# Storing the last block with one transfer per unit, and splitting two units' transposes over several steps, in an attention and feed-forward kernel

## Chip, cores and metric

The kernel runs on 1 core of one Trainium2 chip. The metric is device time in microseconds (us) of one execution; lower is better. TensorE is called PE, VectorE DVE, ScalarE ACT, GpSimd POOL and SyncE SP, as in the profile; SPq and ACTq are the queues on which SP and ACT issue transfers.

## What is computed

```python
def _attn_ref(r, k, v, w, u):              # B=4, H=8, S=768, D=48
    for t in range(S):
        kt, vt, rt = (k[:, :, t], v[:, :, t], r[:, :, t])
        cur = np.einsum('bhd,bhe->bhde', u[None] * kt, vt)
        y[:, :, t] = np.einsum('bhd,bhde->bhe', rt, state + cur)
        state = w[None, :, :, None] * state + np.einsum('bhd,bhe->bhde', kt, vt)
# x = y laid out as 3072 tokens x 384
def _moe_ref(x, w_in, w_out):              # 384 -> 2048 -> 384
    g = np.maximum(x @ w_in, 0.0) ** 2
    return g @ w_out
def _moe2_ref(x, w_a, w_b, w_out):         # 384 -> 1536 -> 384
    return ((x @ w_a) * (x @ w_b)) @ w_out
```

All in float32. Each product of matrices in the two feed-forward layers is made of three passes on PE (high part by high part, high by low, low by high).

## The kernel before

The 3072 tokens are 6 blocks of 512. A block is 4 units of attention (24 in all, numbered `e`); a unit is 2 batches by 64 time steps, 128 rows. The first block's attention is made at the start. From then on the attention of block m is made beside layer 1 of block m-1. Layer 1 of a block has 16 steps; a step's global number is `s = n * 16 + f`. In step s, PE multiplies `up` for step s+2, then does what stands beside the step (a `mix` of a unit, if one is placed there), then `down` for step s. DVE in step s squares the hidden values of step s+2 (`square`), does the placed work, and makes their low part `g_lo` (`square_lo`). All orders are written out by hand: `place` puts units at steps by a table, and each engine's `layer1` asks at each step what stands there.

A unit needs on DVE: its k transposed and scaled (`flip_k`), its r transposed and scaled (`flip_r`), a sum for the diagonal (`sum_diagonal`, for which POOL makes the products), and later `mask` and `keep_state`. Units 8 and up are transposed on DVE; earlier ones on PE. `flip_k` has one buffer `kT`, so it waits until PE has scored the unit before. `mix(e, s)` on PE waits for both scalings of unit e+1, runs `mix_state`, then waits for `g_lo` of step s+1 and scores unit e+1, then runs two more groups.

Before the change, unit 8 is placed at step 8, where unit 6 is mixed: `flip_k` follows `keep_state`, `flip_r` stands at the step's end, and the sum at step 9. Unit 9 is placed at step 13, in which nothing is mixed: `flip_k` and `flip_r` both stand ahead of `square`, and the sum behind it. `mix(8)` stands at step 14.

The kernel's end: in layer 2 of the last block the last step's products finish in four chunks of PSUM, one per 128 tokens, each counted by `chunk_done`. Each chunk is copied to `y_out` in SBUF (128 partitions by 384 floats), chunks 0 and 2 by ACT, 1 and 3 by DVE, and stored by `store_unit`. The 128 partitions of a chunk are 64 tokens of one batch and 64 of another, so its rows lie in two places of the result. SP stores chunks 0, 1 and 2 in this order, ACT chunk 3; each as two transfers of 64 rows. SP then waits for all of them. The stores of the earlier blocks (L480) are 4 transfers of 192 KB each, whose outermost dimension is 64.

Of the kernel before, what the change touches and what calls it, by code (L numbers as in the profile page):

```python
# [28 lines left out]
def attention_ffn_kernel(nc, r, k, v, w, u, w_in, w_down, w_a, w_b, w_out, out):  # L29
# [5 lines left out]
    T = HP  # L35
# [28 lines left out]

    TURN, LATER, FLIP, SCORE, MIX, SPLIT = range(6)
    beside = [{} for _ in range(6)]

    def place(m, turns, later, mixes, splits):  # L70
        for i in range(UNITS):
            e, start = m * UNITS + i, (m - 1) * N1
            beside[FLIP if e >= FLIPPED else LATER if i in later else TURN][start + turns[i]] = e

            assert mixes[i] % 2 == 0
            beside[MIX][start + mixes[i]] = e
            beside[SPLIT].setdefault(start + splits[i], []).append(e)

    beside[SCORE][3] = UNITS
    place(1, [2, 3, 5, 7], [1, 2, 3], [4, 6, 8, 10], [9, 11, 12, 12])  # L80
    for m in range(2, BLOCKS):
        place(m, [-8, -3 if m == 2 else -4, 1 if m == 2 else 0, 4], [], [-2, 2, 6, 10], [5, 6, 12, 12])

    MAIN = 2 * D
# [12 lines left out]
    with ctx:  # L98
# [3 lines left out]
        def sem(name):  # L102
            return ctx.enter_context(nc.semaphore(name))
# [132 lines left out]
        acc_read, x2_stored = sem("acc_read"), sem("x2_stored")  # L236
        x2_loaded = [sem(f"x2_loaded{i}") for i in range(2)]
        up2_done, chunk_done, y_stored = sem("up2_done"), sem("chunk_done"), sem("y_stored")
        even_out, odd_out = sem("even_out"), sem("odd_out")

        def after(eng, signal, count):
            if count > 0:
# [141 lines left out]

        def store_unit(eng, e):

            for i in range(2):
                eng.dma_start(out_t[2 * i + e % 2, LAST, :, e // 2, :], y_out[i * T:(i + 1) * T, e, :])\
                    .then_inc(y_stored, 16)

        block = ctx.enter_context(nc.Block())

        @block.sync
        def _(sp):
            def load_half(e):
                sp.wait_ge(mixed, e - 2)
                load_rk(sp, e, 1, k, k_loaded)
                load_rk(sp, e, 0, r, r_loaded)
                load_v(sp, e)

            def blocks_free(e):

                if e == FLIPPED:

                    sp.wait_ge(scored, UNITS)
                    sp.wait_ge(rest_zeroed, 1)
                    sp.wait_ge(choice_made, 1)
                elif e == FLIPPED + 2:

                    after_split(sp, N1 - 2)  # L410
                    sp.wait_ge(r_flipped, 1)
                elif e == FLIPPED + 4:
                    after_split(sp, N1 - 1)
                else:
                    sp.wait_ge(k_flipped, e - 2 - FLIPPED)
                    sp.wait_ge(r_flipped, e - 2 - FLIPPED)

            def store_x2(n):
                sp.wait_ge(acc_read, (n + 1) * KT)
                sp.dma_start(x2_dram[n, :, :], x2_flat).then_inc(x2_stored, 16)  # L420

            def load_x2(n):
                sp.wait_ge(x2_stored, 16 * (n + 1))
                sp.dma_start(xT[:, n % 2, LO, :, :].rearrange("p k t -> p (k t)").bitcast(F32),
                             x2_dram[n, :, :]).then_inc(x2_loaded[n % 2], 16)

            for e in (0, 2):
                load_rk(sp, e, 1, k, k_loaded)
                load_rk(sp, e, 0, r, r_loaded)
            for e in (0, 2):  # L430
                load_v(sp, e)
            for i in range(2):
                load_weights(sp, i)
            repack(sp, 0)
            for i in range(2, STAGES + 1):
                load_weights(sp, i)

            sp.wait_ge(y_mixed, UNITS)
            load_half(UNITS)
            load_half(UNITS + 2)  # L440
            blocks_free(FLIPPED)
            load_blocks(sp, FLIPPED)

            for n in range(BLOCKS):
                if n > 0:
                    store_x2(n - 1)
                if n < LAST:
                    for e in range((n + 1) * UNITS, (n + 2) * UNITS, 2):
                        repack(sp, e)
                        if e + UNITS < ALL:  # L450
                            load_half(e + UNITS)
                        if e == FLIPPED - 2:
                            blocks_free(FLIPPED + 2)
                            load_blocks(sp, FLIPPED + 2)
                        if FLIPPED + 2 < e + UNITS + 2 < ALL:
                            blocks_free(e + UNITS + 2)
                            load_blocks(sp, e + UNITS + 2)
                if n == LAST - 1:
                    sp.wait_ge(k_flipped, ALL - FLIPPED)
                    sp.wait_ge(r_flipped, ALL - FLIPPED)  # L460
                    for i in range(N1, N1 + STAGES):
                        load_weights(sp, i)

            sp.wait_ge(up_done, N1 * LAST)
            load_x2(0)
            for i in range(N1 + STAGES, N1 + N2):
                load_weights(sp, i)
            sp.wait_ge(up_done, N1 * BLOCKS)
            load_x2(1)
            store_x2(LAST)  # L470

            for n in range(BLOCKS):
                if 1 <= n < LAST:
                    sp.wait_ge(up2_done, n * 2 * N2)
                    load_x2(n + 1)
                if n < LAST:
                    sp.wait_ge(acc_read, BLOCKS * KT + (n + 1) * UNITS)
                    for p in range(2):
                        for i in range(2):
                            sp.dma_start(out_t[2 * i + p, n, :, :, :], y_out[i * T:(i + 1) * T, p::2, :])\  # L480
                                .then_inc(y_stored, 16)

            sp.wait_ge(even_out, 1)
            store_unit(sp, 0)
            sp.wait_ge(odd_out, 1)
            store_unit(sp, 1)
            sp.wait_ge(even_out, 2)
            store_unit(sp, 2)
            sp.wait_ge(y_stored, 16 * (4 * LAST + 2 * UNITS))

        @block.gpsimd
        def _(pool):
# [405 lines left out]
        def _(act):  # L898
# [118 lines left out]
            def take_out(n):  # L1017
                after(act, y_stored, n * 4 * 16)
                if n == 0:
                    act.wait_ge(x2_stored, 16 * BLOCKS)  # L1020
                if n == LAST:

                    for b in (0, 2):
                        act.wait_ge(chunk_done, b + 1)
                        nc.scalar.activation(y_out[:, b, :], acc2[b][:, 0:DM], ACT.Copy).then_inc(even_out, 1)
                    act.wait_ge(odd_out, 2)
                    store_unit(act, 3)
                    return
                act.wait_ge(down_done, STEPS1 + (n + 1) * N2)
                for b in range(UNITS):  # L1030
                    nc.scalar.activation(y_out[:, b, :], acc2[b][:, 0:DM], ACT.Copy).then_inc(acc_read, 1)
# [16 lines left out]
        def _(dve):  # L1048
# [162 lines left out]
            def layer1(n):  # L1211
                for f in range(N1):
                    ahead = (n, f + 2) if f + 2 < N1 else (n + 1, f + 2 - N1) if n < LAST else None
                    s = n * N1 + f

                    flip_first = s in beside[FLIP] and s not in beside[MIX]
                    if flip_first:
                        flip_k(beside[FLIP][s])
                        flip_r(beside[FLIP][s])
                    if ahead:  # L1220
                        square(*ahead)
                    if flip_first:
                        sum_diagonal(beside[FLIP][s])
                    if s - 1 in beside[FLIP] and s - 1 in beside[MIX]:
                        sum_diagonal(beside[FLIP][s - 1])
                    if s in beside[TURN]:
                        sum_diagonal(beside[TURN][s])
                        scale(beside[TURN][s])
# [2 lines left out]
                    if s in beside[MIX]:  # L1231
                        e = beside[MIX][s]
                        if e + 1 < ALL:
                            mask(e + 1)
                        if e < LEAVING:
                            keep_state(e)
                        if s in beside[FLIP]:
                            flip_k(beside[FLIP][s])
                    if ahead:
                        square_lo(*ahead)  # L1240
                    if s in beside[LATER]:
                        scale(beside[LATER][s])
                        sum_diagonal(beside[LATER][s])
# [3 lines left out]
                        x2_lo(0, f - 8)  # L1247
                    for i in split_beside(n, f):
                        split_lo(nc.vector, i)
                    if s in beside[FLIP] and not flip_first:  # L1250
                        flip_r(beside[FLIP][s])

            dve.wait_ge(rest_zeroed, 1)
            for e in range(2):
# [59 lines left out]
                    if n < LAST and 4 <= j < 4 + KT:  # L1314
                        x2_lo(n + 1, j - 4)
            dve.wait_ge(y_stored, LAST * 4 * 16)
            for b in (1, 3):
                dve.wait_ge(chunk_done, b + 1)
                nc.vector.tensor_copy(y_out[:, b, :], acc2[b][:, 0:DM]).then_inc(odd_out, 1)

# [21 lines left out]
```

## Time and profile before

| | |
|---|---|
| median of 3 runs | 918.14 us (917.87 to 919.39) |
| profiled execution, its own time | 918.38 us |
| its span in the trace | 916.6 us |
| PE busy, share of the span | 906.4 us, 99% |
| DVE, ACT, POOL busy | 43%, 31%, 13% |
| DMA, read and written | 38.54 MB and 9.44 MB, mean 52 GB/s |

Times in the trace are from the span's start. The chain of work that ended last is PE for 95% of the span. The tail is what comes after PE's last matmul: copies, issues, data, the landing. The "DMA share" is the mean busy share of 16 DMA engines.
### The profile page before, as it was taken

How to read it: one execution, taken by the hardware profiler on the slowest of the kernel's cores; microseconds unless marked ns; L12 is line 12 of the kernel's file. 1: busy time of each engine (PE TensorE's matmuls, PEld its weight loads, DVE VectorE, ACT ScalarE, POOL GpSimd, SP SyncE). 2: the span in 40 equal slices, each digit the busy share in tenths (PEclk: the TensorE clock that was granted, in tenths of full speed). 3: DMA queues.
4: the chain of work that ended last, by engine and by line, in shares of the span. 5: the costliest groups of instructions: out<-in, count | busy, mean ns of one | idle time of the engine just before them, and what ended most of it. 6: DMA issues, size and time to landing. Idle time of an engine off the chain costs nothing.

```text
span 916.6 us, 16503 instructions
## 1 busy us (share of the span) xinstructions
PE 906.4 (99%) x6951; PEld 774.9 (85%) x6951; DVE 390.8 (43%) x600; ACT 286.0 (31%) x501; POOL 122.7 (13%) x125
## 2 busy tenths in 40 slices
PE   8999999999999999999999999999999999999997
PEld 6888888888888888888888888888888888888886
DVE  8778655546555555336542212322321222222122
ACT  3434333333333233344542222212222222222121
POOL 7355322232223221000000000000000000000000
PEclk9999999999999999999999999999999999999999
DMA  9987536635435320043330001002002002001001
GB/s 154 176 141 144 92 55 118 93 76 86 79 64 92 54 64 20 18 131 120 93 105 1 1 12 59 1 1 70 0 1 69 1 1 69 1 1 34 1 1 35
DMA packets 175800, 53.39 MB, mean 58 GB/s; under 512 B 147949, under 2 KB 174190, under 8 KB 175726
## 3 DMA queue, kind: packets, MB, share of 16 engines
q1 hardware_dynamic: 168832, 47.41, 25.7%
q10 hardware_dynamic: 6894, 4.92, 2.5%
q8 instruction: 55, 0.90, 0.4%
q14 instruction: 19, 0.16, 0.1%
HBM read 38.54 MB, written 9.44 MB: 52 GB/s over the span
## 4 chain that ended last, share of the span: by engine, by line
PE 95%; DVE 1%; issue 1%; POOL 1%; ACT 0%; ACTq 0%; POOLq 0%; DVEq 0%
PE banks L850 11%; PE banks L852 11%; PE banks L851 11%; PE banks L736 7%; PE banks L737 7%; PE banks L740 7%; PE banks L720 7%; PE banks L722 7%; PE banks L721 7%; PE banks L864 5%; PE banks L868 5%; PE banks L865 5%; PE banks L638 1%; PE banks L651 1%; PE banks L618 1%
## 5 line engine op out<-in xcount | busy, mean ns | idle before, releaser
L1298 DVE TENSOR_TENSOR g_raw<-banks,g_raw 128x512 f32<-128x512 f32 x72 | 49.8, 692 | 277.0 <-PE banks L852 277.0
L850 PE MATMUL banks<-xT,weights 128*128 128x512 f32 x360 | 140.2, 389 | 0.0
L851 PE MATMUL banks<-xT,weights 128*128 128x512 f32 x360 | 140.0, 389 | 0.0
L852 PE MATMUL banks<-xT,weights 128*128 128x512 f32 x360 | 140.0, 389 | 0.0
L736 PE MATMUL banks<-g_hi,weights 128*128 128x512 f32 x288 | 114.8, 398 | 0.0
L1183 DVE TENSOR_TENSOR g_lo<-banks,g_hi 128x512 fp32r<-128x512 f32 x94 | 65.1, 692 | 113.1 <-ACT g_hi L912 113.1
L720 PE MATMUL banks<-xT,weights 128*128 128x512 f32 x288 | 112.4, 390 | 0.0
L737 PE MATMUL banks<-g_hi,weights 128*128 128x512 f32 x288 | 112.2, 390 | 0.0
L721 PE MATMUL banks<-xT,weights 128*128 128x512 f32 x288 | 112.1, 389 | 0.0
L722 PE MATMUL banks<-xT,weights 128*128 128x512 f32 x288 | 112.0, 389 | 0.0
L912 ACT ACTIVATE g_hi<-banks 128x512 fp32r<-128x512 f32 x94 | 56.4, 600 | 150.2 <-PE banks L740 107.9
L1012 ACT ACTIVATE g_raw<-banks 128x512 f32<-128x512 f32 x72 | 43.1, 598 | 168.7 <-PE banks L852 168.7
L1015 ACT ACTIVATE g_hi<-g_raw 128x512 fp32r<-128x512 f32 x72 | 45.5, 632 | 160.6 <-DVE g_raw L1298 160.6
L1178 DVE TENSOR_TENSOR banks<-banks,g_raw 128x512 f32<-128x512 f32 x94 | 65.4, 696 | 51.0 <-ACT g_raw L906 50.8
L906 ACT ACTIVATE g_raw<-banks 128x512 f32<-128x512 f32 x96 | 57.4, 598 | 84.9 <-PE banks L722 83.1
L864 PE MATMUL banks<-weights,g_hi 128*128 128x384 f32 x240 | 80.9, 337 | 0.0
L740 PE MATMUL banks<-g_lo,weights 128*128 128x512 f32 x288 | 80.9, 389 | 0.0
L865 PE MATMUL banks<-weights,g_hi 128*128 128x384 f32 x240 | 80.6, 336 | 0.0
L852 PEld LDWEIGHTS banks<-xT,weights 128*128 128x128 f32 x360 | 67.6, 188 | 14.2
L850 PEld LDWEIGHTS banks<-xT,weights 128*128 128x128 f32 x360 | 67.6, 188 | 11.7
L851 PEld LDWEIGHTS banks<-xT,weights 128*128 128x128 f32 x360 | 67.6, 188 | 11.7
L1301 DVE TENSOR_TENSOR g_lo<-g_raw,g_hi 128x512 fp32r<-128x512 f32 x72 | 49.8, 692 | 50.3 <-ACT g_hi L1015 50.3
(131 smaller groups left out, 1246.6 us busy)
## 6 DMA issues: line engine op xcount, KB each, us to landing
rkv<-in_v SPq DMA_DIRECT2D x24, 192.0 KB, 4.4
x_dram<-stage SPq DMA_DIRECT2D x6, 768.0 KB, 3.4
xT<-x_dram SPq DMA_DIRECT2D x6, 768.0 KB, 5.5
result<-stage SPq DMA_DIRECT2D x20, 192.0 KB, 3.0
xT<-y_pad SPq DMA_DIRECT2D x22, 144.0 KB, 2.8
stage<-in_moe_w_out SPq DMA_DIRECT2D x16, 192.0 KB, 3.2
rkv<-in_k SPq DMA_DIRECT2D x12, 192.0 KB, 3.6
rkv<-in_k SPq DMA_DIRECT2D x24, 96.0 KB, 3.6
```

The lines of the kernel that those rows point to most:

```text
L720: nc.tensor.matmul(hid[f % 2][:, :], hi, xT[:, q, HI, kt, :], start=(kt == 0), stop=False)
L721: nc.tensor.matmul(hid[f % 2][:, :], hi, xT[:, q, LO, kt, :], start=False, stop=False)
L722: last = nc.tensor.matmul(hid[f % 2][:, :], lo, xT[:, q, HI, kt, :], start=False, stop=(kt == KT - 1))
L736: nc.tensor.matmul(acc[m][:, :], hi(m), g_hi[:, f % 2, :], start=(f == 0), stop=False)
L737: nc.tensor.matmul(acc[m][:, :], lo(m), g_hi[:, f % 2, :], start=False, stop=False)
L740: last = nc.tensor.matmul(acc[m][:, :], hi(m), g_lo[:, f % 2, :], start=False, stop=(f == N1 - 1))
L850: nc.tensor.matmul(dst, hi, xT[:, q, HI, kt, :], start=(kt == 0), stop=False)
L851: nc.tensor.matmul(dst, hi, xT[:, q, LO, kt, :], start=False, stop=False)
L852: last = nc.tensor.matmul(dst, lo, xT[:, q, HI, kt, :], start=False, stop=(kt == KT - 1))
L864: nc.tensor.matmul(acc2[b][:, 0:DM], p_hi, hi, start=(j == 0), stop=False)
L865: nc.tensor.matmul(acc2[b][:, 0:DM], p_hi, lo, start=False, stop=False)
L1178: nc.vector.tensor_tensor(squared(n, f), squared(n, f), g_raw[:, f % 2, :], ALU.mult)\
```

## The change

Two parts. First, `store_unit` issues one transfer for a unit in place of two; its destination takes both batches by a stride of 2 in the outermost dimension. ACT now copies chunks 0 and 3, DVE chunks 1 and 2, and the last store, by ACT's queue, waits for ACT's own copy. Second, `flip_k`, `flip_r` and the sum get a table each for units 8 and 9: unit 8 has `flip_k` at step 8, `flip_r` and the sum at step 9; unit 9 has `flip_k` at step 10, `flip_r` at step 12, the sum at step 13. Units 10 and up stay where they were.

```diff
+            if e in (FLIPPED, FLIPPED + 1):
+                for kind, at in zip((FLIP_K, FLIP_R, SUM), turns[i]):
+                    beside[kind][start + at] = e
...
-    for m in range(2, BLOCKS):
-        place(m, [-8, -3 if m == 2 else -4, 1 if m == 2 else 0, 4], [], [-2, 2, 6, 10], [5, 6, 12, 12])
+    place(2, [(-8, -7, -7), (-6, -4, -3), 1, 4], [], [-2, 2, 6, 10], [5, 6, 12, 12])
+    for m in range(3, BLOCKS):
+        place(m, [-8, -4, 0, 4], [], [-2, 2, 6, 10], [5, 6, 12, 12])
...
         def store_unit(eng, e):
-            for i in range(2):
-                eng.dma_start(out_t[2 * i + e % 2, LAST, :, e // 2, :], y_out[i * T:(i + 1) * T, e, :])\
-                    .then_inc(y_stored, 16)
+            eng.dma_start(out_t[e % 2::2, LAST, :, e // 2, :], y_out[:, e, :]).then_inc(y_stored, 16)
...
-            sp.wait_ge(even_out, 1)
+            sp.wait_ge(outer_out, 1)
             store_unit(sp, 0)
-            sp.wait_ge(odd_out, 1)
+            sp.wait_ge(inner_out, 1)
             store_unit(sp, 1)
-            sp.wait_ge(even_out, 2)
+            sp.wait_ge(inner_out, 2)
             store_unit(sp, 2)
-            sp.wait_ge(y_stored, 16 * (4 * LAST + 2 * UNITS))
+            sp.wait_ge(y_stored, 16 * (4 * LAST + UNITS))
...
-                    for b in (0, 2):
+                    for b in (0, 3):
                         act.wait_ge(chunk_done, b + 1)
-                        nc.scalar.activation(y_out[:, b, :], acc2[b][:, 0:DM], ACT.Copy).then_inc(even_out, 1)
-                    act.wait_ge(odd_out, 2)
+                        nc.scalar.activation(y_out[:, b, :], acc2[b][:, 0:DM], ACT.Copy).then_inc(outer_out, 1)
+                    act.wait_ge(outer_out, 2)
                     store_unit(act, 3)
...
-                    flip_first = s in beside[FLIP] and s not in beside[MIX]
-                    if flip_first:
+                    if s in beside[FLIP]:
                         flip_k(beside[FLIP][s])
                         flip_r(beside[FLIP][s])
                     if ahead:
                         square(*ahead)
-                    if flip_first:
+                    if s in beside[FLIP]:
                         sum_diagonal(beside[FLIP][s])
-                    if s - 1 in beside[FLIP] and s - 1 in beside[MIX]:
-                        sum_diagonal(beside[FLIP][s - 1])
+                    if s in beside[FLIP_R]:
+                        flip_r(beside[FLIP_R][s])
...
-                        if s in beside[FLIP]:
-                            flip_k(beside[FLIP][s])
+                    if s in beside[FLIP_K]:
+                        flip_k(beside[FLIP_K][s])
                     if ahead:
                         square_lo(*ahead)
+                    if s in beside[SUM]:
+                        sum_diagonal(beside[SUM][s])
...
-                    if s in beside[FLIP] and not flip_first:
-                        flip_r(beside[FLIP][s])
...
-            for b in (1, 3):
+            for b in (1, 2):
                 dve.wait_ge(chunk_done, b + 1)
-                nc.vector.tensor_copy(y_out[:, b, :], acc2[b][:, 0:DM]).then_inc(odd_out, 1)
+                nc.vector.tensor_copy(y_out[:, b, :], acc2[b][:, 0:DM]).then_inc(inner_out, 1)
```

How the instructions of DVE stand from step 12 to step 13, before (L1178 is `square`, L1183 `square_lo`, L1201 the low part of the next block's input, L1139 and L1141 `flip_k`, L1146 and L1148 `flip_r`, L1108 the sum):

```order
L1178 TENSOR_TENSOR banks<-banks,g_raw 128x512
L1183 TENSOR_TENSOR g_lo<-banks,g_hi 128x512
L1201 TENSOR_TENSOR xT<-xT 128x3x128 x2
L1139 STREAM_TRANSPOSE kT<-stage 128x512
L1141 TENSOR_TENSOR kT<-kT,pow_down 112x512
L1146 STREAM_TRANSPOSE rT<-stage 128x512
L1148 TENSOR_TENSOR rT<-rT,pow_up 112x512
L1178 TENSOR_TENSOR banks<-banks,g_raw 128x512
L1108 TENSOR_REDUCE diag<-rku 128x8
L1183 TENSOR_TENSOR g_lo<-banks,g_hi 128x512
```

The same two steps in the changed kernel, whose lines are numbered 5 higher there (L1183 is now `square`, L1188 `square_lo`, L1206 the input's low part, L1151 and L1153 `flip_r`, L1113 the sum):

```order
L1183 TENSOR_TENSOR banks<-banks,g_raw 128x512
L1151 STREAM_TRANSPOSE rT<-stage 128x512
L1153 TENSOR_TENSOR rT<-rT,pow_up 112x512
L1188 TENSOR_TENSOR g_lo<-banks,g_hi 128x512
L1206 TENSOR_TENSOR xT<-xT 128x3x128 x2
L1183 TENSOR_TENSOR banks<-banks,g_raw 128x512
L1188 TENSOR_TENSOR g_lo<-banks,g_hi 128x512
L1113 TENSOR_REDUCE diag<-rku 128x8
```

Unit 9's `flip_k` has left this stretch (it stands at step 10, behind `keep_state`), its `flip_r` has moved up by one step into the place between `square` and `square_lo`, and the sum stands behind `square_lo`.

The end of SP's queue before, with the waits (L388 is in `store_unit`; the sizes are those of the destination, outermost first):

```order
L480 DMA result<-stage 64x2x384 x3
L388 DMA result<-stage 64x384 [waits even_out]
L388 DMA result<-stage 64x384
L388 DMA result<-stage 64x384 [waits odd_out]
L388 DMA result<-stage 64x384
L388 DMA result<-stage 64x384 [waits even_out]
L388 DMA result<-stage 64x384
L98 UNCONDITIONAL_BRANCH [waits y_stored]
```

The same in the changed kernel:

```order
L485 DMA result<-stage 64x2x384 x3
L394 DMA result<-stage 2x64x384 [waits outer_out]
L394 DMA result<-stage 2x64x384 [waits inner_out] x2
L105 UNCONDITIONAL_BRANCH [waits y_stored]
```

Six issues have become three, and the outermost dimension of the destination was 64 and is 2; the source's, the partitions, was 64 and is 128. ACT's queue goes in the same way from two issues of 64x384 to one of 2x64x384. At ACT's start stands the one other transfer with few outermost entries that the text below speaks of, in both kernels:

```order
L968 DMA y_pad<-in_w 4x2x48
L970 DMA y_pad<-in_u 1x384
L972 ACT_TABLE_LOAD
```

The first of these writes 4 partitions with 2 pieces of 48 floats each; it moves nothing between the two kernels.

## Rows read from the trace of the kernel before

**Rows 1.** The page, busy time of the engines, share of the span.

```profile
PE 906.4 (99%) x6951; PEld 774.9 (85%) x6951; DVE 390.8 (43%) x600; ACT 286.0 (31%) x501; POOL 122.7 (13%) x125
```

**Rows 2.** Waits of PE from 60 us on: total us, times, longest.

```profile
PE banks L618 <- DVE g_lo L1183: 0.4, 1, 0.4
```

**Rows 3.** Timeline of PE: start, us, instruction, idle before it.

```profile
95.30 0.39 PE L720 MATMUL banks<-xT,weights 128*128 128x512 f32 x1
...
102.78 0.84 PE L740 MATMUL banks<-g_lo,weights 128*128 128x512 f32 x3
...
106.62 0.69 PE L618 MATMUL banks<-rT,kT 48*64 48x64 f32 x32 [0.36 <-DVE g_lo L1183]
```

**Rows 4.** Timeline of DVE, steps 8 to 13.

```profile
80.65 1.78 DVE L1141 TENSOR_TENSOR kT<-kT,pow_down 112x512 f32<-112x512 f32 x1
...
92.11 0.69 DVE L1183 TENSOR_TENSOR g_lo<-banks,g_hi 128x512 fp32r<-128x512 f32 x1 [1.39 <-ACT g_hi L912]
...
100.28 0.69 DVE L1183 TENSOR_TENSOR g_lo<-banks,g_hi 128x512 fp32r<-128x512 f32 x1 [1.36 <-ACT g_hi L912]
100.88 1.02 DVE L1201 TENSOR_TENSOR xT<-xT 128x384 fp32r<-128x384 f32 x2
101.82 0.71 DVE L1139 STREAM_TRANSPOSE kT<-stage 128x512 f32<-128x512 f32 x1
...
104.52 0.69 DVE L1178 TENSOR_TENSOR banks<-banks,g_raw 128x512 f32<-128x512 f32 x1
...
105.87 0.69 DVE L1183 TENSOR_TENSOR g_lo<-banks,g_hi 128x512 fp32r<-128x512 f32 x1 [0.21 <-ACT g_hi L912]
```

**Rows 5.** Timelines of POOL and of ACT in the same stretch.

```profile
80.88 1.01 POOL L517 TENSOR_TENSOR rku<-rkv,u_rows 128x384 f32<-128x384 f32 x1
...
101.62 0.60 ACT L906 ACTIVATE g_raw<-banks 128x512 f32<-128x512 f32 x1 [0.56 <-PE banks L722]
```

**Rows 6.** Timelines of the last microseconds: ACT and its queue, DVE, SP's queue.

```profile
911.27 0.49 ACT L1025 ACTIVATE stage<-banks 128x384 f32<-128x384 f32 x1 [0.49 <-PE banks L868]
912.38 1.21 ACTq L388 DMA_DIRECT2D result<-stage  x2
...
911.79 0.56 DVE L1319 COPY stage<-banks 128x384 f32<-128x384 f32 x1 [0.42 <-PE banks L868]
...
910.80 3.73 SPq L388 DMA_DIRECT2D result<-stage  x6
```

**Rows 7.** DMA from 911.6 us on, in windows: width, busy engines, PEclk, DMA share, GB/s.

```profile
911.60:912.00 0.40, 0.15 (x1) 0.00 (x0) 0.21 (x1) 0.16 (x1) 0.00 (x0) 1.00 0.11 27
...
915.60:915.80 0.20, 0.00 (x0) 0.00 (x0) 0.00 (x0) 0.00 (x0) 0.00 (x0) 1.00 0.31 100
915.80:916.00 0.20, 0.00 (x0) 0.00 (x0) 0.00 (x0) 0.00 (x0) 0.00 (x0) 1.00 0.00 0
```

**Rows 8.** DMA packets from 910 to 917 us, the eight stores of 64 rows.

```profile
DMA packets 640, 0.79 MB, mean 112 GB/s; under 512 B 128, under 2 KB 640, under 8 KB 640
```

**Rows 9.** DMA to 3.4 us: packets of ACT's queue; the transfer of w, its KB.

```profile
q10 hardware_dynamic: 12, 0.00, 0.3%
...
y_pad<-in_w ACTq DMA_DIRECT2D x1, 1.5 KB
```

**Rows 10.** The four stores of 192 KB of the block before (L480), 843.5 to 848.6 us.

```profile
DMA packets 576, 0.79 MB, mean 154 GB/s; under 512 B 64, under 2 KB 576, under 8 KB 576
...
q1 hardware_dynamic: 576, 0.79, 56.3%
```

**Rows 11.** When SP issued them: start, us for all.

```profile
843.51 2.54 SPq L480 DMA_DIRECT2D result<-stage  x4
```

**Rows 12.** The same stores in windows of 0.4 us, columns as in Rows 7.

```profile
846.20:846.60 0.40, 0.40 (x4) 0.40 (x4) 0.40 (x1) 0.00 (x0) 0.00 (x0) 1.00 0.87 215
...
847.40:847.80 0.40, 0.40 (x4) 0.40 (x4) 0.40 (x1) 0.00 (x0) 0.00 (x0) 1.00 1.01 376
847.80:848.20 0.40, 0.40 (x3) 0.33 (x2) 0.22 (x1) 0.00 (x0) 0.00 (x0) 1.00 0.28 92
```

More of the change, by code:

```diff
@@ L62, in attention_ffn_kernel @@
     assert LATE_SIZE >= LATE * TILE2 and (N2 - LATE) * TILE2 <= N1 * 2 * W1
-    TURN, LATER, FLIP, SCORE, MIX, SPLIT = range(6)
-    beside = [{} for _ in range(6)]
+    TURN, LATER, FLIP, FLIP_K, FLIP_R, SUM, SCORE, MIX, SPLIT = range(9)
+    beside = [{} for _ in range(9)]
     def place(m, turns, later, mixes, splits):
@@ L72, in place @@
             e, start = m * UNITS + i, (m - 1) * N1
-            beside[FLIP if e >= FLIPPED else LATER if i in later else TURN][start + turns[i]] = e
+            if e in (FLIPPED, FLIPPED + 1):
+                for kind, at in zip((FLIP_K, FLIP_R, SUM), turns[i]):
+                    beside[kind][start + at] = e
+            else:
+                beside[FLIP if e >= FLIPPED else LATER if i in later else TURN][start + turns[i]] = e
             assert mixes[i] % 2 == 0
@@ L238, in attention_ffn_kernel @@
         up2_done, chunk_done, y_stored = sem("up2_done"), sem("chunk_done"), sem("y_stored")
-        even_out, odd_out = sem("even_out"), sem("odd_out")
+        outer_out, inner_out = sem("outer_out"), sem("inner_out")
         def after(eng, signal, count):
```

## The prediction

> **What bounds the kernel now.** I read the page first: PE is busy for 906.4 of 916.6 us [rows 1], so a change can only win what PE waits for, or what lies after its last matmul. Then the list of PE's waits from 60 us on, where all of the changed schedule lies: it has one entry, 0.36 us [rows 2, 3]. That is the score of unit 9 inside `mix(8)`, which was ready at 106.26 us and started at 106.62 because `g_lo` of step 15 came late. The timeline of DVE shows why. DVE finished the last work of step 12 late (L1201, 100.88 to 101.9), then put `flip_k` and `flip_r` of unit 9 (101.82 to 104.52, 2.70 us) ahead of `square`, though ACT had the input of `square` ready at 102.22; so `g_lo` started at 105.87 and ended at 106.56 [rows 4, 5]. Last the tail, from timelines and narrow windows: ACT's queue is through with its two issues at 913.59, SP's with its six at 914.53, 3.73 us after the first at 910.80, some 0.62 us each [rows 6]. The first data moves at about 911.9, the last at about 915.8, and the span ends 0.8 us later [rows 7]. The tail is set by SP's issues: chunk 2 is copied at 911.76, but the last issue starts some 2.1 us later [rows 6].
>
> **Part 1, the transposes.** Nothing is added; five instructions of unit 9 and three of unit 8 move. At step 12, `flip_r` of unit 9 falls into DVE's idle 1.36 us between `square` and the `g_lo` of 100.28; a pair of transpose and scaling takes half of 2.70, 1.35 us, so it fits [rows 4]. At step 10, `flip_k` falls into an idle 1.39 us in the same way [rows 4]. At step 13 `square` now starts at about 102.3, and not 104.52; ACT's high part waits for it and for PE's `down` of step 13, which ends at 103.62 [rows 3]; from there `g_lo` is done no later than the 1.35 us by which its start followed `square`'s before, 105.0, some 1.2 us ahead of the score at 106.26. So PE's 0.36 us go. What lies queued behind `flip_k` at step 10 is that step's `g_lo` (92.11); PE needs it for the `up` that starts at 95.30 [rows 3, 4], so 2.5 us of cover. Unit 8 moves its `flip_r` behind `square` instead of ahead of it, which frees `g_lo` of that step and leaves the mix at step 10 on time. Bounds: one scaling of this form took 1.78 us beside POOL's products, against 0.69 as a rule [rows 4, 5]; if `flip_k` at step 10 meets the same, its step is 1.1 us later, inside the cover. So this part is worth between 0 (the lateness is handed on) and 0.4; I take **-0.36 us**.
>
> **Part 2, the stores.** Issues: SP has three in place of six, so its queue is through at about 910.80 + 3 x 0.62 = 912.7, ACT's store is issued at about 912.3 after its own copy of 0.49 us [rows 6]. On its face that takes 1.8 us off SP's queue. But a transfer must be dealt out to DMA engines, and here the shape matters. The stores of 64 rows show 640 packets for 8 transfers: 8 x 64 = 512 of data and 128 of under 512 bytes, which is 16 closing packets for each, so 16 engines [rows 8]. The four stores of 192 KB, whose outermost dimension is 64 too, show 512 + 64, again 16 each [rows 10]. The transfer of w has 4 outermost entries. It is 1.5 KB in pieces of 48 floats (192 bytes), which is 8 packets of data, and there are 12 packets: 4 closing ones, so 4 engines [rows 9]. The trace thus shows that few outermost entries mean few engines. The new stores have 2 outermost entries in the destination and 128 in the source. No row shows a transfer whose two sides differ so. I take it that the smaller side decides, since each engine must be given a whole slice of both sides: **2 engines** for each store, and I take it to be the same two for all four.
>
> The Trainium skill says just this: in "DMA: Bandwidth & Descriptors", section "Why a DMA increments its semaphore by 16 and not by 1", the number of engines is the largest up to 16 that divides the outermost non-1 size of both sides, and they are the lowest-numbered ones. The trace agrees in its three countable cases, none of them with unequal sides.
>
> The price: 4 stores x 128 rows over 2 engines are 256 packets for each engine. A packet's time from the stores of the block before: at their fastest 376 GB/s over 16 engines at a share of 1.01, 1536 x 16 / 376 = 65 ns; in slow windows 215 GB/s, 1536 x 16 / 215 = 114 ns [rows 12]; in the mean 0.563 x 5.1 x 16 / 512 = 90 ns [rows 10]. That one and the same kind of packet takes 65 or 114 ns while all engines are busy says that the slow ones wait for something the 16 share; two engines alone move at most 47 GB/s, so I take the fast end, 65 ns: 256 x 0.065 = **16.7 us** (23.0 at the mean, 29.2 at the slow pace).
>
> **Sum**, in the profiled execution. First data at 911.9 - 0.36 = 911.5; last at 911.5 + 16.7 = 928.2; the span's end 0.8 later, 929.0; against 916.6 that is +12.4. What lies outside the span (918.38 - 916.6 = 1.8 us) stays. The profiled time is 0.24 us above the median of the runs, 918.14, so I add the difference to the median: 918.14 + 12.4 = **930.6 us**. Own range of this case: from 926.4, if ACT's store has engines of its own and SP's three take 3 x 64 x 0.065 = 12.5 us, to 943.1 at 114 ns. I keep 925 to 941, as two lone engines should be nearer to the fast rows. The swapped copies (ACT 0.49 us, DVE 0.56) cost or give less than 0.1 us beside this.
>
> **Rivals.**
> 1. *Sixteen engines all the same* (the side with 128 partitions decides, or the transfer is cut otherwise). For it: the stores whose source has 64 partitions run on 16 [rows 8, 10], and no row tells which side is asked. Then the tail is like the stores of the block before: four transfers of 192 KB issued 0.6 us apart, whose data ended between 847.8 and 848.2, about 4.6 us after the first issue at 843.51 [rows 11, 12]. Here 910.80 + 4.6 = 915.4 against 915.8: -0.4, and up to 0.3 more because ACT issues the fourth at 912.3 beside SP. It would not give the 1.8 us of issue time, since the DMA engines become the bound. With -0.36 that is -0.8 to -1.1: 917.0 to 917.4 us, no change that can be measured (0.2% is 1.8 us here, about what a measurement of this kernel can tell from no change). The Trainium skill's table in "Rules for kernel authors" of the same page even asks for one transfer of 128 partitions in place of two over halves; it takes both to run on all engines, which is this rival. Chance 0.13.
> 2. *Two engines, each queue with its own pair*: 926.4 us as above. Against it: nothing in the trace tells queues' engines apart. Inside the forecast's range, chance 0.05.
> 3. *Two engines at the mean pace or slower*, if the pace is that of writing rows from far-apart partitions and not of sharing: 90 ns give 911.5 + 23.0 + 0.8 - 916.6 = +18.7, so 936.8 us. For it: 90 ns is the mean of the row [rows 10]; against it: two lone engines share with nobody. Chance 0.2, inside the range up to about 108 ns.
> 4. *The schedule makes a new wait*: if a `flip_r` of unit 8 or 9 also took 1.78 us, it would end 1.1 us later; the mix at step 10 would wait up to 0.4 us, an estimate from that 1.1 us less the 0.7 us that I count as cover there. That changes the sum by less than 1 us, and would turn the sign only where the first rival holds and the mix waits over 1.1 us. Chance 0.1, beside any of the others.
>
> **How the numbers follow.** Two engines 0.83 (0.2 of it at a slower pace, 0.05 with pairs apart), sixteen 0.13, a number in between (4 or 8, 920 to 924 us) 0.04. The predicted time is that of two engines at 65 ns. The range 925 to 941 holds 0.83 less 0.03 for a pace above 108 ns: 0.80. Slower by over 0.2%: 0.83 + 0.04 = 0.87, less a little for a number in between that hides, 0.86. Of the sixteen-engine case, 0.11 within 0.2% and 0.03 faster, if both queues overlap better than the row of the block before.
>
> **What would show it.** In the changed kernel's trace: PE without a wait from 60 us on, score of unit 9 at about 106.3; `square` of step 13 at about 102.3. In the tail SPq with three issues ended by 912.7, and then a DMA share of about 2/16 = 0.12 at some 47 GB/s, for 16 to 17 us; 520 packets for the four stores (512 + 8), where sixteen engines would give 576. The long wait would be SP's last, for `y_stored`. The prediction is wrong if the count is 576, and only its size is wrong if the share is 0.12 but the GB/s differ from 47.

## The result, and the profile after

The changed kernel takes 931.18 us in the median of 4 runs (930.15 to 931.94), against 918.0 us before in the same comparison: a ratio of 1.014, 95% interval 1.0122 to 1.0157. The predicted time was 930.6 us, slower with a chance of 0.86.

The page of the changed kernel first, busy time and share of the span, against [rows 1]:

```profile
span 930.2 us, 16499 instructions
...
PE 906.5 (97%) x6951; PEld 774.5 (83%) x6951; DVE 391.6 (42%) x600; ACT 286.1 (31%) x501; POOL 122.4 (13%) x125
```

No engine works longer; the span is 13.6 us longer, and PE's share falls to 97%. So the time lies after PE. The list of SP's waits from 905 us on says where:

```profile
SPq L394 <- ACT stage L1030: 64.7, 1, 64.7
SPq L105 <- DMA result<-stage: 14.3, 1, 14.3
```

The same wait in the kernel before:

```profile
SPq L98 <- DMA result<-stage: 1.7, 1, 1.7
```

The wait at the program's end, for the last stores, is 14.3 us and was 1.7. The timelines of the tail, SP's queue, ACT and its queue, DVE, against [rows 6]:

```profile
911.36 4.09 SPq L394 DMA_DIRECT2D result<-stage  x3
...
912.35 0.49 ACT L1030 ACTIVATE stage<-banks 128x384 f32<-128x384 f32 x1 [1.01 <-PE banks L873]
912.87 0.61 ACTq L394 DMA_DIRECT2D result<-stage  x1
...
911.38 1.02 DVE L1323 COPY stage<-banks 128x384 f32<-128x384 f32 x2 [1.13 <-PE banks L873]
```

The last of the four issues to start is ACT's, at 912.87 us. SP's third starts at 912.60 and takes 2.85 of the 4.09 us, so it ends at 915.45; the two before it took 0.62 and 0.52. The DMA packets from 910 to 931 us, against [rows 8]:

```profile
DMA packets 520, 0.79 MB, mean 37 GB/s; under 512 B 8, under 2 KB 520, under 8 KB 520
...
q1 hardware_dynamic: 390, 0.59, 8.1%
q10 hardware_dynamic: 130, 0.20, 2.5%
```

q1 is SP's queue and q10 ACT's; the numbers are packets, MB and the share of the 16 engines' time. There are 512 rows and 8 closing packets for 4 stores: 2 engines each, where 16 closed each store before. DMA in windows, columns as in [rows 7]:

```profile
914.00:916.00 2.00, 0.00 (x0) 0.00 (x0) 0.00 (x0) 0.00 (x0) 0.00 (x0) 1.00 0.13 38
916.00:918.00 2.00, 0.00 (x0) 0.00 (x0) 0.00 (x0) 0.00 (x0) 0.00 (x0) 0.62 0.13 51
918.00:920.00 2.00, 0.00 (x0) 0.00 (x0) 0.00 (x0) 0.00 (x0) 0.00 (x0) 0.50 0.13 49
...
929.00:929.50 0.50, 0.00 (x0) 0.00 (x0) 0.00 (x0) 0.00 (x0) 0.00 (x0) 0.50 0.12 43
929.50:930.20 0.70, 0.00 (x0) 0.00 (x0) 0.00 (x0) 0.00 (x0) 0.00 (x0) 0.50 0.00 0
```

The share is 0.13, which is 2 of 16 engines. From 918 to 922 us each of the two queues moved 66 packets at this share: the queues share one pair. They move 49 to 51 GB/s: 2 x 1536 bytes each 61 ns. After ACT's copy ends at 912.84 us no engine computes any more; only the issues and the data are left. (The last column but two is the clock granted to PE, whose last matmul ended at 912.3 us. It reads 0.50, the lower of its two levels, from 918 us on.)

From the first issue to the span's end the tail is 930.2 - 911.36 = 18.8 us, before it was 916.6 - 910.80 = 5.8: +13.0 us. The first issue itself comes 0.56 us later than before. To see why, I follow PE's products with `g_lo` (L740 before, L745 after), one group for each step of layer 1. Each row is the group of one step of the changed kernel, 9 to 14:

```profile
85.02 0.84 PE L745 MATMUL banks<-g_lo,weights 128*128 128x512 f32 x3
...
91.25 0.85 PE L745 MATMUL banks<-g_lo,weights 128*128 128x512 f32 x3
...
95.36 0.84 PE L745 MATMUL banks<-g_lo,weights 128*128 128x512 f32 x3
...
99.85 0.84 PE L745 MATMUL banks<-g_lo,weights 128*128 128x512 f32 x3
...
103.93 0.84 PE L745 MATMUL banks<-g_lo,weights 128*128 128x512 f32 x3
...
110.12 0.84 PE L745 MATMUL banks<-g_lo,weights 128*128 128x512 f32 x3
```

The same groups of before start at 84.11, 90.52, 94.62, 98.70, 102.78 and 109.56. So this execution is 0.91 us late at step 9. It was so at step 8 too (80.94 against 80.03 us), ahead of the moved work, so this is the timing of its start. At step 14 it is 0.56 us late. From step 9 to step 14 it takes 25.10 us in place of 25.45: -0.35. Step by step the distances are 6.23, 4.11, 4.49, 4.08, 6.19, and before 6.41, 4.10, 4.08, 4.08, 6.78. Two steps with a mix became shorter, by 0.18 and 0.59 us, and one step longer, by 0.41. From step 14 to the first store both take 801.24 us.

### The profile page after: what moved, and what is told of

It reads as the page before. It is cut to its first block, busy times and chain, and to the rows that moved or that the text cites. A ratio compares the mean times of both kernels' runs of the same rounds, so it can differ in the third digit from the quotient of the medians.

```text
span 930.2 us, 16499 instructions
## 1 busy us (share of the span) xinstructions
PE 906.5 (97%) x6951; PEld 774.5 (83%) x6951; DVE 391.6 (42%) x600; ACT 286.1 (31%) x501; POOL 122.4 (13%) x125
## 4 chain that ended last, share of the span: by engine, by line
PE 92%; SPq 3%; DVE 2%; DMA 1%; issue 0%; POOL 0%; ACT 0%; ACTq 0%; DVEq 0%
PE banks L855 11%; PE banks L857 11%; PE banks L856 11%; PE banks L741 7%; PE banks L742 7%; PE banks L745 7%; PE banks L725 7%; PE banks L726 7%; PE banks L727 7%; PE banks L869 5%; PE banks L873 5%; PE banks L870 5%; PE banks L643 1%; PE banks L656 1%; PE banks L623 1%; SPq L329 1%
## 5 line engine op out<-in xcount | busy, mean ns | idle before, releaser
L1188 DVE TENSOR_TENSOR g_lo<-banks,g_hi 128x512 fp32r<-128x512 f32 x94 | 65.0, 691 | 111.5 <-ACT g_hi L917 111.5
L1183 DVE TENSOR_TENSOR banks<-banks,g_raw 128x512 f32<-128x512 f32 x94 | 65.4, 696 | 51.0 <-ACT g_raw L911 50.8
L745 PE MATMUL banks<-g_lo,weights 128*128 128x512 f32 x288 | 80.9, 389 | 0.0
```

Of the source, the lines that this page charges most:

```text
L745: last = nc.tensor.matmul(acc[m][:, :], hi(m), g_lo[:, f % 2, :], start=False, stop=(f == N1 - 1))
L1183: nc.vector.tensor_tensor(squared(n, f), squared(n, f), g_raw[:, f % 2, :], ALU.mult)\
```

## The experiments

Each ratio is taken to runs of the kernel before that were made beside it; their medians are 918.26 to 918.62 us.

**Each part alone.** Kernel one is that of before with the new end (DVE copies chunks 1 and 2, and the waits follow, as in the change):

```diff
-            for i in range(2):
-                eng.dma_start(out_t[2 * i + e % 2, LAST, :, e // 2, :], y_out[i * T:(i + 1) * T, e, :])\
-                    .then_inc(y_stored, 16)
+            eng.dma_start(out_t[e % 2::2, LAST, :, e // 2, :], y_out[:, e, :]).then_inc(y_stored, 16)
...
-                    for b in (0, 2):
+                    for b in (0, 3):
```

> The kernel before with only the end of the changed kernel: one transfer of 2x64x384 for each unit, chunks 0 and 3 copied by ACT. If the whole loss is from two outermost entries, thus two DMA engines: 520 packets in the four stores, DMA share 0.13 at about 49 GB/s for some 16.9 us, 931.2 us plus or minus 0.8 (the time of the changed kernel, plus up to 0.4 for PE's old wait at the score of unit 9). If part of the loss is from the moved transposes: at least 1 us less than the changed kernel, under 930 us.

Measured: 931.38 us (930.86 to 931.77), 1.0142 of before (1.0126 to 1.0157). 520 packets again; its tail is 929.5 - 910.67 = 18.8 us. PE's wait at the score of unit 9 is there (0.35 us). With the transposes as before the loss is all there: it comes from the new end.

Kernel two has the new tables and `layer1` of DVE, and the stores, copies and waits of before.

> The kernel before with only the moved transposes. If the stores are the whole loss: 917.3 to 918.3 us, same as before. In the trace PE's 0.36 us wait at the score of unit 9 is gone. In the changed kernel PE started the product up for step 14 some 0.4 us late (at 96.28 us), just after DVE's low part of weight tile 14 ended (96.22). If that is caused by the unit's k scaled at step 10 ahead of it, the same gap stands here; if it came from the later start of that execution alone, it doesn't.

Measured: 917.91 us (917.04 to 918.69), 0.9995 of before (0.9985 to 1.0004), no change that can be told. From step 9 to 14 it takes 24.68 us, 0.77 less than before, and no wait of PE is left in the list. Here PE's late start at step 12 was 0.04 us, not 0.41.

**Where the destination lies.** In the changed kernel, only the destination of the four stores differs. This kernel's result is not the right one, as the rows of the last block stand permuted in it; it only answers the question:

```diff
-            eng.dma_start(out_t[e % 2::2, LAST, :, e // 2, :], y_out[:, e, :]).then_inc(y_stored, 16)
+            rows = out.rearrange("(b c t) d -> b c t d", b=B, c=BLOCKS)
+            eng.dma_start(rows[e, LAST, :, :], y_out[:, e, :]).then_inc(y_stored, 16)
```

> The changed kernel, but each of the last four stores writes its 128 rows to one place of the result (128 rows in a row, outermost 128, so that rows of the last block stand permuted in the result). One transfer for a unit stays. If the outermost entries of the destination set the number of engines: 576 packets, all 16 engines, the tail like the four 192 KB stores of the block before, last data some 4.6 us after the first issue, 916.9 to 917.8 us. If one transfer of 128 partitions is slow by itself (many rows behind one issue), it stays near 931 us.

Measured: 916.01 us (915.34 to 916.61), 0.9973 of before (0.9964 to 0.9983). Its packets, and three of its windows, columns as in [rows 7]:

```profile
DMA packets 576, 0.79 MB, mean 30 GB/s; under 512 B 64, under 2 KB 576, under 8 KB 576
...
911.43:911.83 0.40, 0.00 (x0) 0.00 (x0) 0.00 (x0) 0.00 (x0) 0.00 (x0) 1.00 1.03 369
911.83:912.23 0.40, 0.00 (x0) 0.00 (x0) 0.00 (x0) 0.00 (x0) 0.00 (x0) 1.00 1.05 373
912.23:912.63 0.40, 0.00 (x0) 0.00 (x0) 0.00 (x0) 0.00 (x0) 0.00 (x0) 1.00 1.03 365
```

16 closing packets for each store: all engines. With the same source, queues and number of rows, the destination alone makes 15 us. Two things differ in it, the outermost size (128 for 2) and the number of places (1 for 2); the next kernel tells them apart. It also came out 0.9 us under my expectation: it moves at 365 to 373 GB/s, while the first store of 64 rows before, when alone, moved at 207:

```profile
912.00:912.20 0.20, 0.00 (x0) 0.00 (x0) 0.20 (x1) 0.00 (x0) 0.00 (x0) 1.00 0.85 207
```

That is taken up below.

It gives each store 4 places of 32 rows (permuted rows again):

```diff
+            rows = out.rearrange("(b c q t) d -> b c q t d", b=B, c=BLOCKS, q=UNITS)
+            eng.dma_start(rows[:, LAST, e, :, :], y_out[:, e, :]).then_inc(y_stored, 16)
```

> The changed kernel, but each of the last four stores writes 4 places of 32 rows (outermost 4; rows of the last block stand permuted in the result). If the number of engines is that of the destination's outermost entries: 512 + 16 = 528 packets, DMA share about 0.25 at some 98 GB/s, 512 / 4 x 61 ns = 7.8 us of data in place of 15.6, so 922.5 to 924.5 us. If only two places far apart are slow, or any outermost under 16 falls back to two engines, about 931; if it spreads over 16 from four on, about 917.5.

Measured: 923.84 us (923.18 to 924.57), 1.006 of before (1.0045 to 1.0075).

```profile
DMA packets 528, 0.79 MB, mean 30 GB/s; under 512 B 16, under 2 KB 528, under 8 KB 528
...
914.00:916.00 2.00, 0.00 (x0) 0.00 (x0) 0.00 (x0) 0.00 (x0) 0.00 (x0) 0.78 0.27 98
```

4 closing packets for each store, a share of 0.27 and 98 GB/s (88 to 101 in the windows to 921 us): 4 engines, each at about the pace of one of the 2. More places did not make it slower than two places did. The count of engines follows the destination's outermost size through 2, 4 and 128.

**The stores as before, the copies as after.** The changed kernel with `store_unit` in two transfers again.

> The changed kernel with only the stores as before: two transfers of 64 rows for each unit, with the changed copies (chunks 0 and 3 by ACT, 1 and 2 by DVE). If the shape of the stores is the whole loss: SP has six issues again, its last starts about 3.1 us after the first, 640 packets, 917.4 to 918.2 us, same as the run of the moved transposes alone (917.9). If the swapped copies cost something by themselves, it is over 918.5.

Measured: 917.96 us (917.4 to 918.91), 0.9993 of before (0.9984 to 1.0002). Its packets are 640 again. The swapped copies cost and give nothing that can be told.

**The new gap on PE.** The chain of waits of the changed kernel around step 12, start, us, what ("issue" is time in which the engine waited for nothing that the profile shows):

```profile
91.54 0.54 DVE state L1177
92.08 0.63 DVE kT L1144
92.71 0.02 issue
92.73 1.79 DVE kT L1146
94.52 0.60 DVE g_lo L1188
95.12 1.11 DVE weights L389
96.23 0.04 issue
96.28 0.50 PE banks L725
```

PE's `up` for step 14 waits for the low part of weight tile 14 (L389, `split_lo`), which stands behind `g_lo` in step 10 and so behind `flip_k` of unit 9. The scaling there took 1.79 us, beside POOL's products. PE could have started at about 96.04 (its group of step 11 at 95.36, plus the 0.68 us after which the next one starts elsewhere). So the start is 0.24 us late; the products behind it take the other 0.17 of the 0.41 us. The experiment takes the transposes alone and moves `flip_k` by one step:

```diff
-    place(2, [(-8, -7, -7), (-6, -4, -3), 1, 4], [], [-2, 2, 6, 10], [5, 6, 12, 12])
+    place(2, [(-8, -7, -7), (-5, -4, -3), 1, 4], [], [-2, 2, 6, 10], [5, 6, 12, 12])
```

> The moved transposes alone, with unit 9's k transposed and scaled at step 11 in place of step 10, beside the same stores as before. Theory: at step 10 the scaling runs beside POOL's products (1.8 us), pushes DVE's low part of weight tile 14 to within 0.1 us of PE's due time or past it, and so costs 0.0 to 0.4 us, by how the execution falls. At step 11 POOL is at its last product: PE's starts of the g_lo products stand 4.08 us apart from step 11 to 12 in every execution, 917.4 to 917.9 us, at most 0.4 below the moved transposes alone. Rival: the gap comes from something else ahead of step 12, and stays.

Measured: 917.59 us (916.88 to 921.64), 0.9996 of before (0.9986 to 1.0006). In time this is not told from either. In the trace the groups stand 4.08 us apart from step 10 to 13, and step 9 to 14 takes 24.62 us; the scaling, at 95.31, took 0.77 us. One trace would not show much here, since the gap comes and goes with `flip_k` at step 10. All traces of this case together show more. With `flip_k` at step 10 there are eight; the scaling took 1.78 to 1.80 us in each, and the distance from step 11 to 12 is 4.10 to 4.12 us in four of them and 4.26, 4.36, 4.49 and 4.51 in the others. With `flip_k` at step 11 there are two, and it is 4.08 in both. The gap's cause is shown by the traces; that it costs time is not resolved by the runs.

**A version that beats both.** One transfer for each unit on all engines needs a destination in one piece. So the tokens of the last block are put in order of batches when layer 2 loads them; `store_unit` writes one place as above, ACT waits for four loads in place of one, and every row of the result stands where it belongs:

```diff
+                if n == LAST:
+                    by_batch = xT[:, n % 2, LO, :, :].bitcast(F32).rearrange("p k (i q s t) -> p k i q s t", i=2, q=2, s=2)
+                    by_unit = x2_dram[n, :, :].rearrange("p (k s q i t) -> p k i q s t", k=KT, s=2, q=2, i=2)
+                    for s in range(2):
+                        for q in range(2):
+                            sp.dma_start(by_batch[:, :, :, q, s, :], by_unit[:, :, :, q, s, :])\
+                                .then_inc(x2_loaded[n % 2], 16)
+                    return
```

> The changed kernel, with the tokens of the last block put in order of batches when layer 2 loads them (four transfers of 128x6x64 in place of one, loaded long before they are used), so that each chunk is 128 rows in one place of the result, every row where it belongs. One transfer of 128x384 for each unit. If the destination's outermost entries are all: like the permuted rows, 576 packets at over 320 GB/s, 915.5 to 916.6 us. If the finer loads (256 bytes a piece) delay layer 2, PE shows a wait at the last block's first product and the gain is smaller.

Measured: 915.63 us (915.36 to 916.0), 0.9967 of before (0.9954 to 0.9979). Its tail, in SP's and ACT's queues:

```profile
909.64 1.44 SPq L395 DMA_DIRECT2D result<-stage  x3
...
911.15 0.38 ACTq L395 DMA_DIRECT2D result<-stage  x1
```

The tail is 913.6 - 909.64 = 4.0 us, against 5.8 before. PE's list shows no wait from 60 us on, so the finer loads are hidden.

> The kernel with chunks by batch, and unit 9's k at step 11 as well. 915.2 to 916.4 us, 0 to 0.4 us below the one with chunks by batch alone; the best version of both changes together, about 0.25% under the kernel before.

Measured: 915.91 us (915.21 to 916.08), 0.9969 of before (0.9957 to 0.9981): inside the expected range, but not below the kernel above. Moving k to step 11 gives nothing that these runs can tell; here step 10 to 11 took 4.22 us, 0.14 more than the plain 4.08, whose cause is not known.

**Why 128 rows move faster than 64.** Both kernels send each unit in two transfers of 64 rows to one place, as permuted rows; one takes partitions 0 to 63 and 64 to 127, the other every second partition:

```diff
+            for i in range(2):
+                eng.dma_start(rows[e, LAST, i * T:(i + 1) * T, :], y_out[i * T:(i + 1) * T, e, :])\
+                    .then_inc(y_stored, 16)
...
+            for i in range(2):
+                eng.dma_start(rows[e, LAST, i::2, :], y_out[i::2, e, :]).then_inc(y_stored, 16)
```

> Each unit in two transfers of 64 rows again, from partitions 0 to 63 and 64 to 127, but to one place of 128 rows (rows of the last block stand permuted in the result). The question is why 128 rows in one transfer moved at 321 to 373 GB/s and took 3.97 us from first issue to the span's end, where the stores before moved at some 207 GB/s when alone and took 5.8. Theory A, a transfer from half of the partitions is slow by its source: it stays at 200 to 230 GB/s when alone, tail 5.7 us, 917.4 to 918.4 us. Theory B, two places of the result far apart are slow: over 320 GB/s, and the tail is set by six issues of 0.4 to 0.6 us, 4.8 to 5.6 us.

> The same with the two transfers of a unit made of every other partition (64 rows each, over all 128 partitions; rows permuted in the result as before). Theory A: pace of the whole, over 320 GB/s when alone, each transfer's packets at 65 ns; the tail is set by six issues, 4.8 to 5.5 us. If any transfer of 64 rows is slow, whatever its partitions: 200 to 230 GB/s and 5.7 us, as with the halves.

Measured: 917.68 us (0.9995 of before, 0.9985 to 1.0004) for the halves and 917.5 us (0.999, 0.9981 to 0.9999) for every second one. The shares of the two queues over 8 us, and the first window of data, in which the first store is alone; first the halves:

```profile
q1 hardware_dynamic: 480, 0.59, 26.6%
q10 hardware_dynamic: 160, 0.20, 10.7%
...
912.17:912.57 0.40, 0.00 (x0) 0.00 (x0) 0.00 (x0) 0.28 (x1) 0.00 (x0) 1.00 0.88 207
```

Then every second partition, with its fastest window:

```profile
q1 hardware_dynamic: 480, 0.59, 20.7%
q10 hardware_dynamic: 160, 0.20, 6.9%
...
911.93:912.33 0.40, 0.00 (x0) 0.00 (x0) 0.00 (x0) 0.28 (x1) 0.00 (x0) 1.00 0.63 223
913.93:914.33 0.40, 0.00 (x0) 0.00 (x0) 0.00 (x0) 0.00 (x0) 0.00 (x0) 1.00 0.93 334
```

A packet takes 0.373 x 8 x 16 / 512 = 93 ns from half of the partitions and 0.276 x 8 x 16 / 512 = 69 ns from all of them. Alone, the first store moves 207 GB/s at a share of 0.88 in the one and 223 at only 0.63 in the other. So the slow packets come neither from 64 rows as such nor from the distance of the places. The second kernel also spreads its rows over every second row of the destination, so this pair alone does not tell source from destination; the stores of the block before do: each wrote 128 neighbouring rows from one half of the partitions, and took 90 ns for a packet [rows 10], where the kernel with the rows in one place wrote such rows from all partitions in (0.207 + 0.068) x 8 x 16 / 512 = 69 ns. It is the half in the source that is slow. The tails are 5.7 and 5.6 us: with six issues of 0.6 us on SP's queue the faster packets hardly help. The second came out 0.1 us over the 4.8 to 5.5 that I had expected.

## Why the prediction was right, step by step

**The number of engines**, the step that carried the sign: right, 2 for each store, and one pair for both queues (rival 2 is out: the share is 0.13 with both under way, 66 packets each from 918 to 922 us). What the trace of before could not show, unequal sides, is shown by the runs: with 128 entries in the source, the destination's 2, 4 or 128 decide 2, 4 or 16. The Trainium skill's rule ("DMA: Bandwidth & Descriptors", "Why a DMA increments its semaphore by 16 and not by 1") agrees with all of it; that the engines are the lowest-numbered ones no row shows. Its other rule ("Rules for kernel authors" of the same page), one transfer over 128 partitions in place of two halves, held here with the rows in one place (916.0 us) and failed with two places (931.2).

**The price.** I took 65 ns for a packet and 16.7 us of data. Measured, the data run for about 16.9 us, but otherwise composed: on each engine a packet starts every 61 ns, 256 x 0.061 = 15.6, and some 1.3 us are lost at the beginning, where the pair moves 12 to 38 GB/s in the windows from 912 to 916 us. The pair thus moves up to 51 GB/s, where I had said at most 47; the slow beginning was not in my sum. That the two errors all but cancel is luck. The argument for the fast end held (rival 3 is out): the slow packets of before were slow by their source in half of the partitions; I had only said that they wait for something that the 16 engines share.

**Part 1.** The sum was right (-0.36 predicted, -0.35 in the profiled execution) by luck, as two errors cancel. In the seven other traces with `flip_k` at step 10, step 9 to 14 is 0.21 to 0.80 us shorter than before. First, the mixes gained more. In PE's timeline of the changed kernel, the first two groups of the mix at step 14:

```profile
106.74 0.67 PE L643 MATMUL banks<-rT,state 48*48 48x64 f32 x32
107.22 0.65 PE L623 MATMUL banks<-rT,kT 48*64 48x64 f32 x32
```

They start 0.48 us apart when nothing is late, though the first shows as 0.67 us busy. The idle time that a row shows starts only behind that, so the wait at step 14 was 0.59 us and not the 0.36 shown, and the mix at step 10 hid another 0.18 without a row in the list. Second, "what lies queued behind `flip_k` at step 10 is that step's `g_lo`" left out the work behind `g_lo`: the low part of weight tile 14, due at the same `up`. Before, it ended at 94.60 us, so the cover was 0.7 us and not 2.5. (Before, it was this very operation that ran beside POOL's products and took 1.76 us; in the changed kernel the scaling did, and it took 1.17.) Its lateness cost 0.41 us here, 0.04 in the kernel with the transposes alone. I had the 1.78 us of the scaling as a bound; it came true, 1.79, and I had wrongly put it inside the cover.

**Issues.** SP was to be through at 912.7; its third issue took 2.85 us and ended at 915.45. It didn't matter, as the pair was busy anyway.

**The other rivals.** A new wait did come (rival 4), but from another instruction than I had named, and it changed no sign; my sign that PE would show no wait was a poor one, as PE's list is empty and the 0.41 us are there: the profile has them as a wait of PE's weight load (0.5 us). The rival of sixteen engines was priced too dear: 917.0 to 917.4 against 916.0 measured. I took the pace from the four stores of 192 KB, whose sources are halves too. The time of 916.0 us is that of permuted rows; with the rows where they belong it is 915.6, and this needed the new order of the loads.

## What to carry to other kernels

Count the 4-byte closing packets of a transfer: they tell how many DMA engines it had. When merging two transfers into one, look at the outermost size of both sides; a small one undoes the merge, and a change of order upstream, where there is time, can give the merged one a destination in one piece. When an operation moves up in an engine's queue, follow all that is queued behind it up to its next idle time, not only the next instruction.

## What the runs showed of the hardware

- Stores of the result whose source is 64 neighbouring partitions move packets of 1536 bytes in 93 ns in the mean; from every second of 128 partitions, 69 ns; from all 128, 69 ns.
- A transfer of 128x384 is issued in 0.34 to 0.38 us, one of 64x384 in 0.49 to 0.61, one of 2x64x384 in 0.52 to 0.63, apart from SP's third.
- With the stores on one pair of engines, the third issue of SP took 2.85 us (2.86 in the kernel with the new end alone). With 4 engines for each store the longest took 0.64. What the long one waits for no row shows.
- The scaling of 112x512 on DVE took 1.78 to 1.80 us in all eight traces in which it stood at step 10 beside POOL's products, 0.77 and 1.07 in the two with it at step 11.
- The start differs by execution: step 9 of layer 1 came at 83.6 to 85.1 us with the same work ahead of it. A gain of 0.3 us in the schedule is read from distances within a trace, not from the time, and from several traces: step 9 to 14 of one schedule took 24.65 to 25.24 us.
